# A mixing, gating and rational layer on one core: two tiles' softmax joined, the fourth tile's exponential and the second layer's weight splits moved

## What is computed

```python
# causal mixing: softmax over 7 taps, for each token and head
w = exp(weight_gen - max(weight_gen, axis=-1))
w = w / (sum(w, axis=-1) + 1e-9)
out[b, s, h, :] = sum over k of w[b, s, h, k] * x_pad[b, s + k, h, :]
# first layer, 192 -> 1536 -> 192
gate = 1 / (1 + exp(-(x @ w_gate)));  val = x @ w_val;  y = gate * val @ w_out
# second layer, 192 -> 2048 -> 192
h = y @ w_in
P = a0 + a1*h + a2*h**2 + a3*h**3
Q = 1 + |b0|*|h| + |b1|*h**2
z = (P / (Q + 1e-6)) @ w_out2
```

## Time and profile before

| | |
|---|---|
| median of 3 runs | 1420.21 us (1420.18 to 1420.8) |
| profiled execution | 1422.31 us, span 1420.4 us |
| TensorE busy | 1379.2 us, 97% of the span |
| VectorE, ScalarE, GpSimd busy | 1259.2, 1083.4, 356.2 us |
| mean granted TensorE clock | 0.993 |
| chain that ended last | PE 90%, DVE 6%, ACT 2%, issue 2% |

### The profile page before, as it was taken

How to read it: one execution, slowest core, us unless ns; L and a number is a source line. 1 busy time by engine, 2 the same in 40 slices (tenths; PEclk the granted TensorE clock), 3 DMA queues, 4 the chain that set the end, 5 groups by cost and what they waited for, 6 DMA issues and landing times.

```text
span 1420.4 us, 19056 instructions
## 1 busy us (share of the span) xinstructions
PE 1379.2 (97%) x7282; PEld 1238.5 (87%) x7282; DVE 1259.2 (89%) x1504; ACT 1083.4 (76%) x1470; POOL 356.2 (25%) x204
## 2 busy tenths in 40 slices
PE   6899999999999999999999999999999999999976
PEld 5789888888889889889889889889898898889966
DVE  7677989999989989889999989899898898889998
ACT  3387887877777788787787777787787778778975
POOL 0143323231332313233131332323233141210000
PEclk9999999999999999999999999999999999999989
DMA  9100100101010010100101010010100001000000
GB/s 242 59 32 1 38 0 1 42 1 43 1 43 1 1 43 1 43 1 0 43 1 43 0 43 1 0 43 0 42 1 29 11 1 34 1 12 0 12 0 17
DMA packets 13468, 33.06 MB, mean 23 GB/s; under 512 B 1601, under 2 KB 7747, under 8 KB 13377
## 3 DMA queue, kind: packets, MB, share of 16 engines
q1 hardware_dynamic: 13312, 31.85, 7.2%
q0 software_dynamic: 64, 0.00, 0.0%
HBM read 25.55 MB, written 6.29 MB: 22 GB/s over the span
## 4 chain that ended last, share of the span: by engine, by line
PE 90%; DVE 6%; ACT 2%; issue 2%; DMA 0%; SPq 0%; DVEq 0%
PE ring L319 49%; PE acc L346 39%; PE ring L373 1%; PE ring L376 1%; DVE work L712 1%; DVE work L719 1%; DVE work L733 1%; DVE work L706 1%; DVE u L700 1%; DVE work L742 0%; DVE work L726 0%; DVE work L653 0%; DMA window<-in_x_dram 0%; ACT work L485 0%; ACT work L487 0%
## 5 line engine op out<-in xcount | busy, mean ns | idle before, releaser
L346 PE MATMUL acc<-out_w,work 128*128 128x192 f32 x2048 | 366.3, 330 | 14.6 <-DVE work L742 14.6
L346 PEld LDWEIGHTS acc<-out_w,work 128*128 128x128 f32 x2048 | 342.5, 193 | 21.4 <-DVE work L742 15.0
L484 ACT ACTIVATE work<-ring,coef 128x512 f32<-128x512 f32 (+1 forms) x272 | 182.2, 670 | 223.9 <-PE ring L319 221.4
L319 PE MATMUL ring<-yt,in_w 128*128 128x512 f32 (+1 forms) x1360 | 330.8, 389 | 2.4 <-DVE work L712 1.9
L346 PE MATMUL acc<-out_w,u 128*128 128x192 f32 x1536 | 284.8, 327 | 6.3 <-DVE u L700 6.3
L319 PEld LDWEIGHTS ring<-yt,in_w 128*128 128x128 f32 x1360 | 245.7, 189 | 51.4 <-DVE work L712 2.9
L319 PE MATMUL ring<-xt,gate_w 128*128 128x512 f32 (+1 forms) x1020 | 267.5, 392 | 3.4 <-DVE work L712 2.1
L346 PEld LDWEIGHTS acc<-out_w,u 128*128 128x128 f32 x1536 | 256.7, 190 | 13.5 <-DVE u L700 7.2
L319 PE MATMUL ring<-xt,val_w 128*128 128x512 f32 (+1 forms) x1020 | 257.0, 382 | 0.0
L603 POOL TENSOR_TENSOR mixed<-mixed,prod 128x768 f32<-128x768 f32 (+1 forms) x90 | 196.7, 2186 | 169.9 <-DVE u L700 150.7
L598 POOL TENSOR_TENSOR prod<-window,mixw 128x768 f32<-128x768 f32 (+1 forms) x90 | 135.0, 1500 | 408.3 <-DVE work L719 307.1
(11 more groups left out here) (57 smaller groups left out, 921.1 us busy)
## 6 DMA issues: line engine op xcount, KB each, us to landing
window<-in_x_dram SPq DMA_DIRECT2D x14, 960.0 KB, 4.6
out_dram<-zsb SPq DMA_DIRECT2D x15, 384.0 KB, 2.5
out_w<-in_moe_w_out_dram SPq DMA_DIRECT2D x1, 1536.0 KB, 19.1
mixw<-in_weight_gen_dram SPq DMA_DIRECT2D x13, 112.0 KB, 2.9
out_w<-in_moe_w_out_dram SPq DMA_DIRECT2D x2, 576.0 KB, 8.7
work<-in_moe_w_in_dram SPq DMA_DIRECT2D x2, 512.0 KB
work<-in_moe_w_in_dram SPq DMA_DIRECT2D x4, 256.0 KB, 13.4
window<-in_x_dram SPq DMA_DIRECT2D x1, 768.0 KB, 4.3
```

The lines of the kernel that those rows point to most:

```text
L319: last = nc.tensor.matmul(dst, wt[:, c], xs[:, 0:n], start=at == 0, stop=at == 4)
L346: last = nc.tensor.matmul(dst, src[:, n * P:(n + 1) * P], w[:, i, :], start=i == 0 and n % 2 == 0, stop=i == last_i and n % 2 == 1, skip_g ...
L484: nc.scalar.activation(den(n), h, ACT.Abs, scale=coef[:, 6:7])
```

## The change

Three things. Tiles 1 and 2 get one softmax: each step runs once over the weights of both, at tile 1's places, and tile 2's own are gone; the steps of all later tiles count one softmax less. The exponential of tile 3 moves from the middle of quarter 6 to the end of quarter 4, behind the third sigmoid, its first two VectorE steps to the middle of quarter 4 and its last four to quarter 5. Pieces 12 to 14 are split at the end of quarter 3, around the split of tile 1's x, and only piece 15 stays in quarter 4, behind its first sigmoid and gating.

```diff
+        def softmax(c):
+            if c == 2:
+                return 1, BLOCKS[1] + BLOCKS[2], mixw[:, 2 * CW - BLOCKS[1] * HK:3 * CW]
+            return max(c - 1, 0), BLOCKS[c], weights(c)
...
             def exponential(c):
-                v = weights(c)
-                act.wait_ge(s_soft, 6 * c + 2)
+                i, _, v = softmax(c)
+                act.wait_ge(s_soft, 6 * i + 2)
                 nc.scalar.activation(v, v, ACT.Exp).then_inc(s_softexp, 1)
...
-            exponential(1)
+            exponential(2)
...
                 if k == 4:
-                    for c in range(12, 14):
-                        split_high(c)
+                    split_high(15)
...
-                if k == 4:
-                    for c in range(14, 16):
-                        split_high(c)
-                if k == 4:
-                    exponential(2)
-                if k == 6:
-                    exponential(3)
...
                 sigmoid(m + 2)
-                if k % 4 == 0 and k > 7:
+                if k % 4 == 0 and k > 3:
                     exponential((k + 1) // 4 + 2)
                 rsqrt(q)
                 if k == 3:
+                    split_high(12)
                     x_twice(1)
                     x_high(1)
+                    split_high(13)
+                    split_high(14)
...
-                pool.wait_ge(s_soft, 6 * (c + 1))
+                pool.wait_ge(s_soft, 6 * c)
...
-            soft(1, 0)
-            soft(1, 1)
+            soft(2, 0)
+            soft(2, 1)
```

More of the change, by code:

```diff
@@ L109, in moe_kernel @@
         mixw = sb("mixw", [P, FIRST * CW])
-        top = sb("top", [P, J * H])
-        total = sb("total", [P, J * H])
+        top = sb("top", [P, OFFS[3] * H])
+        total = sb("total", [P, OFFS[3] * H])
         mixed = sb("mixed", [P, J, D])
@@ L610, in soft @@
                     return
-                n = BLOCKS[c] * H
-                w3 = weights(c).rearrange("p (n k) -> p n k", k=K)
-                base = 6 * c
+                i, blocks, w = softmax(c)
+                n, base = blocks * H, 6 * i
+                w3 = w.rearrange("p (n k) -> p n k", k=K)
                 def over_k(v):
@@ L627, in soft @@
                 elif step == 2:
-                    dve.wait_ge(s_softexp, c + 1)
+                    dve.wait_ge(s_softexp, i + 1)
                     nc.vector.reduce_sum(total[:, 0:n], w3, AX_X).then_inc(s_soft, 1)
@@ L772, in _ @@
                 if k == 4:
-                    for c in range(12, 14):
-                        split_low(c)
+                    split_low(15)
                 quotient(p - 3)
-                if k % 4 == 1 and k > 8:
+                if k % 4 == 1 and k > 4:
                     for step in range(2, 6):
@@ L784, in _ @@
                     for step in range(2, 6):
-                        soft(1, step)
+                        soft(2, step)
                 if k == 1:
@@ L797, in _ @@
                 if k == 4:
[L798 to L803, removed]
                     soft(3, 0)
@@ L831, in _ @@
                     early_mix(4, 1)
[L832 to L837, removed]
                 quadratic(n + 3)
@@ L843, in _ @@
                 if k == 3:
+                    split_low(12)
                     x_low(1)
+                    split_low(13)
+                    split_low(14)
         @block.gpsimd
```

## The result

The changed kernel takes 1399.15 us (median of 4, 1397.49 to 1399.94) against 1420.51 us (4 runs, 1420.18 to 1421.82): ratio 0.9845, 95% interval [0.9829, 0.9860]. I had forecast 1411.7 us, range 1409.2 to 1416.0. The direction was right and the size was not: 21.4 us gained for 8.5.

The account below looks back on a forecast made before the run. TensorE's own stream was taken to bound 97 to 1320 us, with only earlier stops removable. 5.0 + 0.33 + 4.2 - 1.0 = 8.5 us less turned the median 1420.21 into 1411.7 us; range 1409.2 to 1416.0.

Parts of the forecast that it names:

- The step that failed: Between 97 and 1320 us TensorE waits 0.3 us in all, so only gains or losses made before about 97 us count.
- My sign of being wrong: If the shift at 100 us is 8.5 us but the end's is not, the tail was misread.
- The first part: Joined softmax's longer instructions from 17.5 us: unit 2 0.66 us later, then 0.35 to 0.45 more; 1.0 us lost.
- rival 1: Clock falls early as TensorE's idle 0.91 us at 20.2 us grows to 1.56; costs 1.9 us, 1413.6 us; chance 0.12.
- The first stop: At 59.75 us TensorE's second product waits 3.09 us for unit 14's u, slow matmuls after; removing it gains 5.0 us.
- Quarter 6: 0.33 us from a stop at 78.18 us, and 84.23 to 96.87 us shortened from 12.64 to 8.46: 4.2 us gained.
- the stop of up to 0.5 us: In quarter 6, a possible remaining stop from late release of two banks by the cubic of units 6 and 7.
- The fourth tile's exponential: Behind unit 14's sigmoid, done with table loads by 60.9 us, before unit 15's sigmoid, which cannot start before 62.2 us.
- The splits: Second layer's weight casts and subtractions fit idle gaps from about 45 to 54 us: no cost, 0.3 us at most.
- GpSimd: Third tile's mixing from 53.9 us meets VectorE's subtraction at 55.5 us, counted at 1.8 us (0.4 to 1.9), but hidden.
- Rival 3: VectorE's subtraction at 55.5 us waits until GpSimd pauses at 63.9 us; only 0.6 us gained, 1419.6 us; chance 0.06.
- The tail: After 1320 us, unedited, assumed unchanged; the shift can add or remove one low-clock loss of 1.8 us.

Follow-up runs that it names:

- e2: Changed kernel with enlarged top and total at the end of memory and an old-size placeholder, so all other buffers keep old addresses: 1412.32 us, ratio 0.9937 to the original.
- e1: Original kernel with 384 unused bytes per partition between total and mixed, moving everything behind up; no instruction moved: 1407.29 us, ratio 0.9898.
- g3: Changed kernel at old addresses, with the splits back in quarter 4; joined softmax and moved exponential kept: 1414.42 us, ratio 0.9962 to the original.
- g2: Changed kernel at old addresses, with the fourth tile's exponential back in quarter 6; joined softmax and spread splits kept: 1416.62 us, ratio 0.9975 to the original.
- g1: Changed kernel at old addresses with only the joined softmax; exponential back in quarter 6, splits in quarter 4: 1416.57 us, ratio 0.9981 to the original.
- f3: Original kernel with 384 unused bytes ahead of the weight tiles and 128 behind the weights, moving the weights only: 1409.54 us, measured once.
- i1: Original kernel with pads placing weights at 0 and xt, yt at 384 in a row of 512 bytes: 1422.62 us, measured once.
- f2: Original kernel with 256 unused bytes ahead of xt and 256 behind yt: 1420.79 us, measured once.
- e3: Original kernel with 384 unused bytes behind yt, moving x_pair, u, work and others but not xt, yt: 1418.25 us, measured once.
- e4: Original kernel with 384 unused bytes ahead of xt and 128 behind yt: 1410.60 us, measured once.
- f1: Original kernel with 128 unused bytes ahead of xt and 384 behind yt: 1411.15 us, measured once.
- i2: Original kernel with 192 unused bytes ahead of xt and 320 behind yt: 1412.42 us, measured once.

## Why the prediction was wrong, step by step

**The step that failed** is the first one: "there the time is TensorE's own stream, and nothing that VectorE, ScalarE or GpSimd do a little earlier or later is worth anything". That is true of their order, and e2 bears it out: with the old addresses the forecast of 1411.7 us met 1412.3 (1411.0 to 1412.9). But I took the pace of that stream as given, 232 ns from pass to pass, and it became 227. The enlarged `top` and `total` moved xt, yt, u and work by 384 bytes, a part of the diff that my sum put at nothing without a reason, and 13.1 of the 21.4 us are that (e1, e2). A sum over instructions and waits could not have found it, and no rival covered it. My sign of being wrong did come up, a shift of 7.95 us near 97 us and of 22.3 at the end, but it would have sent me to the tail, which is worth 1.2 us of the difference; the stream between is worth 13.2. So the right direction is owed to the forecast's own terms, and the size beyond them to something that it did not have.

**The first part** (1.0 us lost early). Unit 2's gate starts 5.90 us behind unit 0's instead of 5.25 (22.85 less 17.60): 0.65 for 0.66. Behind it, g3, at full clock, needs 23.80 us from there to the x transposes, before 23.36: 0.44 for "0.35 to 0.45". 1.1 us for 1.0, right. In the changed kernel's profiled execution rival 1 added about 1 us to it (24.85 against g3's 23.80), not the 1.9 that I gave it; e2, g2 and g3 show no low clock behind this stop, g1 does, with nearly the same stops (1.57 and 1.56 us in g1 and g3). In e2 and g2 unit 0 itself starts 0.5 us later than before, at 18.09, and that is why their x transposes are 1.46 us late; behind unit 0 they lose 1.0.

**The first stop** (5.0 us). Gone, with its low clock, and the size is right: from the x transposes to unit 15's value side before takes 20.84 us (46.21 to 67.05), e2 15.84 (47.67 to 63.51). What took it away is the end of tile 2's own softmax, as g1 shows; my working credited the splits' spread beside it, which for this stop was worth nothing.

**Quarter 6** (0.33 and 4.2 us). The sizes are right: the stretch took 12.64 us before and takes 8.47 in e2 (80.23 to 88.70), the 0.33 us ahead of it came as 0.43 (from the second products at 76.55 us to unit 18's gate 2.90 us before, 2.47 in e2), and the stop of up to 0.5 us that I left possible did not stay. The parts are not: I put 1.7 of the 4.2 us down to the low clock. From unit 20's gate to unit 21's it is 7.06 us with the low clock (before, f3, i1) and without it (e1, g2, f2). At full clock TensorE waits for u instead (1.11 us in g2), and unit 21's gate waits for its bank in both (0.31 and 0.48 us), so the low clock cost nothing here.

**The fourth tile's exponential** at the end of quarter 4: right, with 1.30 us to spare in front of unit 15's sigmoid. **The splits**: cost nothing, as forecast (x transposes to unit 12's gate 3.2 us before and in e2), and without their spread this place has a stop of 1.72 us (g3).

**GpSimd**: the subtraction took 0.53 us, not 1.8, hidden either way. In g3 it took 1.42 and helped to make a stop. Rival 3 did not happen in either.

**The tail** came out 1.2 us shorter, within the 1.8 us that I allowed for one low clock; one of its three low clocks falls elsewhere:

```profile
1362.03 2.87 PE L352 MATMUL acc<-out_w,work 128*128 128x192 f32 x16 [1.91 <-DVE work L743]
...
1379.22 2.93 PE L352 MATMUL acc<-out_w,work 128*128 128x192 f32 x8 [3.02 <-DVE work L743]
...
1388.13 7.15 PE L352 MATMUL acc<-out_w,work 128*128 128x192 f32 x32 [3.33 <-DVE work L743]
```

The stop of 1.9 us is no longer followed by slow matmuls (2.87 us for sixteen, 4.55 before), the one of 3.0 us now is (2.93 for eight, 1.57 before), and the last stop is 3.33 instead of 4.28 us. One slip of the working: the range begins at 1409.2 us and the bounds ahead of it at 1409.5, and the text gives no reason for the difference; nothing hangs on it.

## What to carry to other kernels

A change that resizes a buffer moves every buffer allocated behind it, and its time contains that move; to read what the edit itself does, keep the addresses (a placeholder in the old place, the new buffer at the end) and time both. Where an engine is busy all the time, ask whether its pace is its best: compare the start-to-start time of equal instructions between versions, and not only its idle time. And an exponential between sigmoids belongs where the engine's next input is late anyway; two of them joined were worth 3.5 us here (g1), after about 1 us that the longer instructions cost.

## What the runs showed of the hardware that I had not expected

- The pace of float32r matmuls of 512 columns depends on where their operands lie relative to each other. With weights and streamed operand 128 bytes apart modulo 256, passes follow at 232 ns, 64 apart at 229, at the same place at 227 to 229 (nine layouts: before, e1, e3, e4, f1, f2, f3, i1, i2). The rest goes with the operands of the second products: 83.65 us to a tile with u and its weights at the same place too, 83.91 with them 128 bytes apart. The 192-column float32 passes themselves stay at 162.5 ns in all of them. Why, and whether u counts by its distance to the weights or to xt, is open.
- The granted clock after a stop is not settled by the stop: at the same place and with stops alike to 0.01 us, g1 fell to 0.50 and g3 did not. Times of one kernel spread by 2 to 5 us and go with the clock of the execution (e1: 1404.29 at 0.996 to 1408.66 at 0.993). Of 21 executions of before beside g1, the 8 with a clock of 0.998 took 1417.5 to 1417.9 us, the others 1419.5 to 1422.3. So e3's 1418.25, a single time at 0.998, is no gain.
- A low clock need not cost anything: behind the stop of 1.74 us in quarter 6 it came in some kernels and not in others, and the next 7.06 us were the same.
- A VectorE instruction with two inputs in memory can slip in between two of GpSimd's at a price of 0.14 us (0.53 for 0.39), with GpSimd's next one 0.15 longer (1.69 for 1.54), or wait 1.0 us for the first of them (1.42), as its start falls.
